# Attention in a routed transformer block: the last step's scores directly behind those of the step before, on one Trainium2 core

## What is computed

```python
scores = scale * np.matmul(q, k.transpose(0, 1, 3, 2))     # 4 x 8 heads, 576 positions, 64 wide
mask = block_i >= block_j                                   # blocks of 64 positions
attn = softmax(np.where(mask, scores, -1e9))
x = np.matmul(attn, v)                                      # back to 2304 tokens x 512
x = (h - np.tanh(h)) @ w_out                                # h = x @ w_in, 512 -> 2048 -> 512
y = gate * (np.maximum(xc @ w1[e], 0) @ w2[e])              # 8 experts, one for each chosen token
```

## Time and profile before

| | before |
|---|---|
| median of 3 runs | 791.15 us |
| lowest, highest | 790.19, 792.12 us |
| the profiled execution, its own time | 790.21 us |
| its span in the profile | 788.5 us |
| PE busy | 772.7 us (98%) |
| DVE, ACT, POOL busy | 500.2, 296.3, 248.7 us |
| granted TensorE clock, mean | 0.998 of full |

### The profile page before, as it was taken

The page is one execution under the profiler, slowest core; times in us unless marked ns, Lnnn a source line. Parts: engine busy times, 40 slices in busy tenths (PEclk is TensorE's granted clock), DMA queues, the critical chain, the costliest instruction groups (busy, mean ns, idle before and its releaser), DMA issues.

```text
span 788.5 us, 14905 instructions
## 1 busy us (share of the span) xinstructions
PE 772.7 (98%) x4600; PEld 605.7 (77%) x4601; DVE 500.2 (63%) x1238; ACT 296.3 (38%) x738; POOL 248.7 (32%) x305
## 2 busy tenths in 40 slices
PE   6999999999999999999999999999999999999996
PEld 3556555655888888888888888889998888888885
DVE  5788788876443367665676566754558465666653
ACT  4777676765110220113101221012227164554642
POOL 4766767676860000002000200002221323333333
PEclk9999999999999999999999999999999999999999
DMA  9253444421337410001000010000172476565563
GB/s 197 63 118 89 98 108 119 102 60 39 109 67 2 102 73 0 1 1 54 0 0 0 0 54 1 0 1 1 54 202 79 125 252 207 198 201 196 177 223 139
DMA packets 88154, 69.27 MB, mean 88 GB/s; under 512 B 66962, under 2 KB 66962, under 8 KB 88104
## 3 DMA queue, kind: packets, MB, share of 16 engines
q1 hardware_dynamic: 83192, 62.93, 30.0%
q0 software_dynamic: 3696, 5.38, 2.1%
q10 hardware_dynamic: 1216, 0.30, 0.2%
HBM read 62.97 MB, written 8.84 MB: 91 GB/s over the span
## 4 chain that ended last, share of the span: by engine, by line
PE 73%; DMA 14%; issue 5%; DVE 3%; POOL 2%; POOLq 1%; ACT 0%; SPq 0%; DVEq 0%
PE psum L1382 49%; DMA xg<-out_dram,rec_next 7%; PE psum L1330 7%; PE psum L1352 6%; PE psum L1301 6%; DMA out_dram<-y_rows,rec_now 4%; PE psum L1283 2%; DMA out_dram<-y_rows,rec_early 2%; PE psum L1429 1%; DVE neg_max L914 1%; POOL rec_next L641 1%; PE psum L1490 1%; DVE we L1227 1%; PE psum L1433 1%; POOLq L395 0%
## 5 line engine op out<-in xcount | busy, mean ns | idle before, releaser
L812 ACT ACTIVATE g<-psum 128x512 f32<-128x512 f32 (+1 forms) x80 | 44.5, 556 | 306.8 <-PE psum L1382 306.8
L1114 DVE TENSOR_TENSOR g<-psum,g 128x512 f32<-128x512 f32 (+1 forms) x80 | 51.1, 638 | 157.5 <-ACT g L812 157.3
L596 POOL DMA_INDIRECT lists<-rec,slot_i x18 | 19.2, 1069 | 331.0 <-DVE slot_i L1052 327.1
L571 POOL TENSOR_SCALAR probs<-probs,row_inv 128x384 f32<-128x384 f32 (+2 forms) x96 | 99.0, 1042 | 54.9 <-DVE row_inv L921 54.9
L1382 PE MATMUL psum<-x_hi,wi_hi 128*128 128x512 f32 x256 | 100.1, 391 | 0.0
L1382 PE MATMUL psum<-x_hi,wi_lo 128*128 128x512 f32 x256 | 99.7, 389 | 0.0
L1382 PE MATMUL psum<-x_lo,wi_hi 128*128 128x512 f32 (+1 forms) x256 | 99.6, 389 | 0.0
L714 ACT ACTIVATE probs<-psum,neg_max 128x576 f32<-128x576 f32 (+2 forms) x144 | 74.6, 527 | 33.8 <-DVE neg_max L914 32.4
L1144 DVE TENSOR_TENSOR we<-w_half,we x96 | 59.0, 685 | 33.5 <-ACT we L696 33.5
L696 ACT ACTIVATE we<-w_half (+1 forms) x112 | 60.1, 620 | 31.1 <-PE psum L1581 27.8
L914 DVE TENSOR_REDUCE neg_max<-psum 128x1 f32<-128x576 f32 (+2 forms) x144 | 63.0, 484 | 13.6 <-PE psum L1330 13.6
(11 more groups left out here) (237 smaller groups left out, 1491.7 us busy)
## 6 DMA issues: line engine op xcount, KB each, us to landing
w_half<-in_moe_w_dram SPq DMA_DIRECT2D x64, 512.0 KB, 4.2
out_dram<-x_rows SPq DMA_DIRECT2D x18, 256.0 KB, 2.1
q_rows<-in_q_dram SPq DMA_DIRECT2D x30, 144.0 KB, 3.0
k_rows<-in_k_dram SPq DMA_DIRECT2D x30, 144.0 KB, 3.2
v_rows<-in_v_dram SPq DMA_DIRECT2D x32, 128.0 KB, 2.3
w_raw<-in_moe_w_in_dram SPq DMA_DIRECT2D x16, 256.0 KB, 3.6
w_raw<-in_moe_w_out_dram SPq DMA_DIRECT2D x16, 256.0 KB, 2.5
wide_x<-w_rows SPq DMA_DIRECT2D x4, 256.0 KB, 5.4
```

Of the source, the lines that this page charges most:

```text
L571: pool.tensor_scalar(p, p, row_inv[:, j, m:m + 1], None, ALU.mult).then_inc(short_normed, 1)
L1114: dve.tensor_tensor(g_f, h_at(f, first, last), g_f, ALU.subtract).then_inc(g_done, 1)
```

## The change

In PE's queue alone, for pairs 1 to 15, the scores of step 3 move ahead: they stood behind T0, and now stand directly behind the scores of step 2, ahead of the weighted sums of the pair before. All other work keeps its order. PE's work of a pair is so in eleven groups of one kind where it was in twelve. Pair 0 keeps its order.

```diff
                 if u > 0:
+                    score(u, 3)
                     weigh_many(u - 1, (2, 3, 4))
                 turn_first(u, 0)
                 turn_second(u, 0)
-                score(u, 3)
-                if u > 0:
+                if u == 0:
+                    score(u, 3)
+                else:
                     weigh_few(u - 1)
                 turn_first(u, 1)
                 turn_second(u, 1)
```

## The result

The changed kernel takes 794.62 us (median of 5 runs, 794.47 to 796.4), the kernel before 791.63 us (5 runs, 790.19 to 792.12). The ratio is 1.0046, with a 95% interval of 1.0035 to 1.0057: slower by 3.6 us (2.8 to 4.5). The forecast was slower, by 5.3 us.

A forecast was written before the change was run, and what follows sets the result against it. PE looks fully busy, but POOL's block 6, hanging on T0, was taken to release it with 0.04 us of room. 0.40 + 5.04 - 0.13 = 5.3 us takes 791.15 to 796.4 us; range 794.6 to 798.2.

The forecast's parts named there:

- The equal 0.11 us between POOL's end and the load: Before T2's second half: 0.11 us from POOL's end to PE's load in pairs 0 and 9, taken as POOL releasing PE.
- the chain: From T0 through DVE's copy, maxima and reciprocal to POOL's block 6 and T2's second half; 5.19 us from T0 to S1.
- the room of 0.04 us: Slack per pair before PE waits for POOL: block 6's end to S1 takes 0.70 us when PE waits, 0.74 in pair 9.
- T0 later, and the rows of DVE and POOL rigidly with it: T0 starts 0.40 us later; DVE's copy and maxima, the reciprocal and POOL's block 6 move equally, row lengths unchanged.
- The merge of S2 and S3, 0.09 us: On PE, scores directly behind scores save 0.09 us a pair: 1.01 less the 0.92 read from S0.
- The bound of 0.18: Upper bound of the merge's saving, if T0's end before Wf, now sums rather than scores, saves as much again.
- The sum: Whole slowdown of 5.3 us: 0.40 in pair 1, 0.36 in each of pairs 2 to 15, less 0.13 in the last.
- X: The start of T0 in a pair, from which the prediction measures times; in pair 1 forecast 0.40 us late.
- Nothing gives it back behind the attention: In the dense layers and experts after the pairs, the 5.3 us delay stays in full.
- A: Rival: PE's work alone sets the time, so only the merge counts; 1.4 us less, 789.8 us; chance 0.05.
- B: Rival: POOL's block 6 gets shorter by 0.3 us without DVE's overlap; +1.1 us, 792.3 us; chance 0.04.
- C: Rival: PE's new idle time draws further waits, 0.1 us more a pair; 6.8 us slower, 798.0 us; chance 0.10.

## Why the prediction was right, and where a term was off

*What bounds the kernel.* Right. The equal 0.11 us between POOL's end and the load was no chance: lengthening the chain by 0.26 us showed the room of 0.04 us, shortening it gave nothing.

*T0 later, and the rows of DVE and POOL rigidly with it.* Right in kind: 4.48 us from T0 to block 6's end, and 5.18 to S1 (5.19 forecast). The size was off, by the next point.

*The merge of S2 and S3, 0.09 us.* This is the term that was mis-sized. S2 and S3 together take 117.60 - 116.27 = 1.33 us, forecast 0.92 + 0.49 = 1.41; before they took 1.01 + 0.49 = 1.50. The merge saves 0.17 us. Where it does so, the start of S3's 192-column product tells, since it runs on the same quarters as the 512-column one. A count of PE's matmuls by shape shows it in the stretch from 117.07 to 117.18 us, and not yet in the one to 117.15:

```profile
L1330 PE MATMUL psum<-kt,qt 64*64 64x192 f32 x1 | 0.3, 323 | 0.0
```

So S2's start to the 192-column product is 117.18 - 116.27 = 0.91 us: the 0.92 taken from S0 was right within 0.01, and the junction saves 0.10. What failed is the other term, S3's own 0.49, which the sum carried over unchanged with no reason given. From the 192-column product to the sums it is now 117.60 - 117.18 = 0.42 us, 0.07 less. Each product stands in the trace as two passes. The first pass of the 192-column product takes 0.21 us to the start of the second where S3 stands behind transposes (116.93 to 117.14), and 0.16 behind other scores (117.18 to 117.34); the other 0.02 lies between the second pass and the next group. Why a first pass behind another kind of work is longer, no run here tells.

One difference between S0 and S3 I had not looked at: the 64-column products of S0 wait for the semaphore `five_scored`, given when the 384-column product beside them is done, and the load's row carries a wait of 0.72 for PE's own product. It mattered little. From the 512-column product's second pass to the product behind it on the same quarters it is 0.44 us in S0 and 0.43 in the changed kernel. The bound of 0.18 that I had given was for another reason (T0's end before Wf), which saved no more than 0.01: T0 to Wf is 108.46 - 107.44 = 1.02, and T0 to S3 was 1.03.

*The sum.* A pair costs 11.44 - 11.16 = 0.28 us and not 0.36. With the measured merge: X of pair 1 later by 0.49 - 0.17 = 0.32, 14 pairs at 0.282 are 3.95, and the last pair's Wm(0,1) gave back 0.12 (0.13 forecast). That is 4.15 us, which the traces show, and 5.3 minus 15 times 0.08 is 4.1.

*The range.* The bounds were 794.6 to 798.2 us, and the median of 794.62 lies inside by 0.02; that of the changed kernel's second set of runs, 794.51, would not. That is luck. The lower bound had allowed the merge 0.15 us, although the part on the merge gave 0.18 as its bound; with the measured 0.17 the forecast of 796.4 would have been 795.2. The terms named, 795.5 and 797.8 with 1 us for the runs, also give 794.5 and 798.8 rather than the bounds stated.

*Nothing gives it back behind the attention.* Right within 0.2 us.

*The rivals.* A fell to the four traces in which PE's own work does set the pace, all at 10.99 or 11.16 us: the bound was there, but only with the chain out of the way. The gain that it would have brought is 2.5 us rather than 1.4, by the same mis-sized term. B: POOL's block 6 has kept its 1.70 us, within 0.01, in each trace that multiplies it whole. C did not come in the changed kernel; ACT's copy behind T1 ended at X + 3.64 and T2 started at X + 3.71, as closely as computed and without cost. Only in the last pair did PE's wait for ACT ahead of T2 grow, from 0.6 to 1.1 us, and there the wait for POOL that follows decides: from T0 to the first dense product it is 5.01 us in both kernels.

## What to carry to other kernels

An engine that is busy all the time may be let go by another at every turn, with no wait on the page. Before moving a group of its work later, list who waits for the group, follow that queue in order to where it comes back, and compare the load's start with the releaser's end against a place where the wait is real. A move on one engine's queue wants the same move on the queues that consume it: here the merge of two groups cost 4.15 us alone and gave 2.5 us once DVE's or ACT's order followed. And a group's length is no constant that can be carried to another place in the order: S3 took 0.49 us behind transposes and 0.42 behind scores, and a term carried over unchanged needs a reason like any other.

## What the hardware showed beyond that

Scores on different quarters of the array pass each other, so that strict order, as told above of an engine's queue, does not hold among them. The program issues step 3's products as 192, 128 and 64 columns, behind 512 and 448. A count of PE's matmuls by shape in a stretch 0.8 us behind the start of S2 (117.07 to 117.15) in the changed kernel shows the 128-column ones running and no 192-column one yet:

```profile
L1330 PE MATMUL psum<-kt,qt 64*64 64x512 f32 x2 | 0.6, 589 | 0.0
L1330 PE MATMUL psum<-kt,qt 64*64 64x448 f32 x2 | 0.5, 536 | 0.0
L1330 PE MATMUL psum<-kt,qt 64*64 64x128 f32 x2 | 0.3, 269 | 0.0
```

The 128-column products use the quarters of the 448-column ones, which come free first: the 448-column second pass starts at 116.71, the 512-column one at 116.75. The passing is hardly what the merge saves. The products of 512 and then 192 columns, which follow each other on the other quarters in the order of the program, take 0.91 and 0.42 us, the whole 1.33 of the merged group. No run here forbids the passing, so what it is worth by itself is not shown.
